# FFT filter and two MLPs on one core: six of sixteen units turned by 64x64 products, filters in places of their own, and the last reload cut in two

## What is computed

```
X = rfft(x, axis=1); y = irfft(X * (filt_r + 1j * filt_i), n=3008, axis=1)
x = y.reshape(6016, 256)
h = x @ w1_in;  x = max(0.01 * h, h) @ w1_out        # 256 -> 2048 -> 256
h = x @ w2_in;  out = max(h, 0)**2 @ w2_out
```

## Time and profile before

| | |
|---|---|
| median of 3 runs | 1065.8 us (1065.09 to 1067.39) |
| the profiled execution | 1064.64 us, of which the span is 1062.5 us |
| PE busy | 1057.0 us, 99% of the span |
| DVE, ACT, POOL busy | 827.9, 563.3, 316.1 us |
| granted TensorE clock | 1.00 of full speed throughout |
| DMA | 61.45 MB, 58 GB/s over the span, 79% of the share from 20 to 90 us |

### The profile page before, as it was taken

One profiled execution on the slowest core, in us unless ns is written; L12 is line 12 of the kernel. 1 busy time (PEld: TensorE's weight loads), 2 busy tenths in 40 slices (PEclk: granted clock), 3 DMA queues, 4 the chain that ended last, 5 costly groups with the idle time before them and its releaser, 6 DMA issues.

```text
span 1062.5 us, 13988 instructions
## 1 busy us (share of the span) xinstructions
PE 1057.0 (99%) x5120; PEld 879.8 (83%) x5120; DVE 827.9 (78%) x1142; ACT 563.3 (53%) x979; POOL 316.1 (30%) x287
## 2 busy tenths in 40 slices
PE   9999999999999999999999999999999999999998
PEld 9558888888888888888999888888888888888998
DVE  2877898887887887787887886887887887786666
ACT  3667564564554654555554554644554554454543
POOL 1995654434343343341321211220220220210000
PEclk9999999999999999999999999999999999999999
DMA  9696000121112112112344000100100100100100
GB/s 316 176 304 231 10 1 17 36 52 46 51 49 49 52 47 51 52 33 55 118 152 147 21 1 1 40 1 1 40 1 1 40 1 1 40 1 1 40 1 35
DMA packets 66724, 61.45 MB, mean 58 GB/s; under 512 B 40688, under 2 KB 53856, under 8 KB 66656
## 3 DMA queue, kind: packets, MB, share of 16 engines
q1 hardware_dynamic: 66160, 60.06, 18.2%
q10 hardware_dynamic: 496, 0.49, 0.1%
HBM read 36.55 MB, written 23.99 MB: 57 GB/s over the span
## 4 chain that ended last, share of the span: by engine, by line
PE 98%; DMA 1%; SPq 0%; DVE 0%; ACT 0%; issue 0%; ACTq 0%
PE PS L1046 16%; PE PS L1047 16%; PE PS L1048 16%; PE PS L1054 14%; PE PS L1055 14%; PE PS L1056 14%; PE PS L935 2%; PE PS L959 2%; PE PS L1002 1%; PE PS L1022 1%; PE PS L979 1%; DMA X<-in_x 0%; DMA zu<-U 0%; DMA V<-zu 0%; SPq L219 0%; PE PS L999 0%
## 5 line engine op out<-in xcount | busy, mean ns | idle before, releaser
L683 ACT ACTIVATE GH<-GF 128x512 fp32r<-128x512 f32 (+1 forms) x384 | 238.7, 622 | 295.3 <-DVE GF L878 154.4
L884 DVE TENSOR_TENSOR GL<-GF,GH 128x512 fp32r<-128x512 f32 (+1 forms) x384 | 273.7, 715 | 110.4 <-ACT GH L683 103.7
L1048 PE MATMUL PS<-GH,WOL 128*128 128x512 f32 (+1 forms) x768 | 295.8, 385 | 0.0
L1047 PE MATMUL PS<-GL,WOH 128*128 128x512 f32 (+1 forms) x768 | 295.8, 385 | 0.0
L1046 PE MATMUL PS<-GH,WOH 128*128 128x512 f32 (+1 forms) x768 | 295.8, 385 | 0.0
L1054 PE MATMUL PS<-XH,WIH 128*128 128x512 f32 (+1 forms) x672 | 259.5, 386 | 0.0
L1056 PE MATMUL PS<-XH,WIL 128*128 128x512 f32 (+1 forms) x672 | 258.8, 385 | 0.0
L876 DVE SCALAR_TENSOR_TENSOR GF<-GF 128x512 f32<-128x512 f32 (+1 forms) x192 | 167.5, 913 | 1.6
L1048 PEld LDWEIGHTS PS<-GH,WOL 128*128 128x128 f32 x768 | 144.2, 188 | 27.0
L1046 PEld LDWEIGHTS PS<-GH,WOH 128*128 128x128 f32 x768 | 144.2, 188 | 26.8
L1047 PEld LDWEIGHTS PS<-GL,WOH 128*128 128x128 f32 x768 | 144.2, 188 | 26.6
(11 more groups left out here) (85 smaller groups left out, 941.9 us busy)
## 6 DMA issues: line engine op xcount, KB each, us to landing
V<-zu SPq DMA_DIRECT2D x12, 512.0 KB, 5.9
zu<-U SPq DMA_DIRECT2D x31, 192.0 KB, 3.7
out_y<-YT SPq DMA_DIRECT2D x5, 1024.0 KB, 4.3
X<-in_x SPq DMA_DIRECT2D x8, 512.0 KB, 8.9
FL<-in_filt SPq DMA_DIRECT2D x16, 224.0 KB, 5.0
wi<-PWH SPq DMA_DIRECT2D x16, 224.0 KB, 2.5
wi<-PWL SPq DMA_DIRECT2D x16, 224.0 KB, 3.1
WIH<-wi SPq DMA_DIRECT2D x8, 448.0 KB, 3.4
```

Of the source, the lines that this page charges most:

```text
L683: nc.scalar.activation(GH[:, g, 0:width(s)], GF[:, g, 0:width(s)], ACT.Copy).then_inc(g_hi[kind], 1)
L884: nc.vector.tensor_tensor(GL[:, g, 0:w], GF[:, g, 0:w], GH[:, g, 0:w].bitcast(f32), ALU.subtract).then_inc(g_lo[kind], 1)
L1047: nc.tensor.matmul(acc, wh, xl, start=False, stop=False)
L1048: return nc.tensor.matmul(acc, wl, xh, start=False, stop=last)
```

## The change

1. **Turn by quarters.** In units 4, 6, 8, 10, 12 and 14 (`by_quarters`), the turn is no longer 8 transposes but 32 ordinary products with the 64x64 identity: for each sequence and frequency, two halves of the feature rows times two halves of the output columns (rows 0 to 47 and 64 to 111 of the result). Bank 0 now takes the first 64 features and bank 1 the last 64, for both sequences, so ACT copies only once all of it is done. In those units the turn stands ahead of `spectrum` in the pass.
2. **Filters.** Each of the 16 filters has a place of its own, ten of them (FLA) in WIH's room behind group 1, six (FLB) where FL was. SP no longer waits for DVE to load them, and loads the weight groups w1i 3 to 6 earlier. In return the rounding of group 2 moves on DVE to behind the last copy of U, and its sums on POOL from units 8 and 11 to behind the units, together with group 3's.
3. **V's second half.** Rows 0 to 95 (units 8 to 13) are loaded by ACT in three DMAs once those units are stored, right behind `x_round0(1)`; rows 96 to 127 (units 14 and 15) by SP in three DMAs once all is stored. The pieces are 4, 8 and 12 of 24 column groups.
4. **PE's order.** `up_1(1)` moves to right behind `up_1(0)`, ahead of sequence 12.

```diff
+V_PIECES = ((0, 4), (4, 12), (12, 24))
+V_BODY = 96
-FSLOTS = 6
+F_EARLY = 10
...
+        def by_quarters(i):
+            return i >= 4 and i % 2 == 0
...
             def load_filter(i):
-                if i >= FSLOTS:
-                    sp.wait_ge(prod, 3 * (i - FSLOTS + 1))
-                elif i == 0:
+                if i == F_EARLY:
                     for half in range(2):
                         sp.wait_ge(n1_ps[half], CH // 2)
...
+            for n in range(3):
+                sp.wait_ge(p_ps, 4 * n + 4)
+                load_filter(6 + n)
+                if n < 2:
+                    load_w1i(3 + n)
             for i in range(UNITS):
-                if i + FSLOTS < UNITS:
-                    load_filter(i + FSLOTS)
                 store_u(i)
-                if i in (1, 2, 4, 6):
-                    load_w1i(WI_EARLY + (1, 2, 4, 6).index(i))
+                if 9 + i < UNITS:
+                    load_filter(9 + i)
+                if i in (1, 2):
+                    load_w1i(4 + i)
...
             for n in range(UNITS - RINGS, UNITS):
                 sp.wait_ge(*stored(n))
-            for g in range(MH // 4):
-                load_v(1, g)
+            for n in range(len(V_PIECES)):
+                load_v_rest(n)
...
-                if i in (8, 11):
-                    wi_sums(2, (8, 11).index(i))
...
+            for k in (2, 3):
+                for part in range(2):
+                    wi_sums(k, part)
             for part in range(3):
-                wi_split(WI_EARLY - 1, part)
-            for k in range(WI_EARLY, WI_SEAM):
+                wi_split(2, part)
+            for k in (4, 5, 6):
                 for part in range(2):
                     wi_sums(k, part)
...
             def turned(i):
+                if by_quarters(i):
+                    act.wait_ge(s2_ps, turned_steps(i + 1))
+                    for h in range(2):
+                        nc.scalar.activation(S2[:, i % 2, :, :, 64 * h:64 * h + 64].rearrange("p b j d -> p (b j) d"),
+                                             PS[0:KR, h, :].rearrange("p (n d) -> p n d", d=64), ACT.Copy).then_inc(s2_sb, 1)
...
             def wi_round(k):
                 act.wait_ge(wi_s, 4 * k + 4)
+                act.wait_ge(wi_hi, k)
...
                 if c == 4:
                     x_round0(1)
+                    for n in range(UNITS - 2 - RINGS, UNITS - 2):
+                        act.wait_ge(z_out[n % RINGS], 32 * (n // RINGS + 1))
+                    for n in range(len(V_PIECES)):
+                        load_v_body(n)
...
-            wi_round(WI_EARLY - 1)
             back(UNITS - 2)
             dve.wait_ge(yf_sb, 2 * UNITS)
             y_copy(1)
             back(UNITS - 1)
+            wi_round(2)
...
+                        for h in range(2):
+                            d = slice(64 * h, 64 * h + 64)
+                            c = 64 * (UJ * b + k)
+                            for part in range(2):
+                                mm = nc.tensor.matmul(PS[IM * part:IM * part + R, h, c:c + 64], TT1[half][d, b, q + part, 0:R],
+                                                      DM[d, 2, d], start=True, stop=True)
...
             for i in range(UNITS):
+                if i + 3 < UNITS and by_quarters(i + 3):
+                    turn(i + 3)
                 if i + 2 < UNITS:
                     spectrum(i + 2)
-                if i + 3 < UNITS:
+                if i + 3 < UNITS and not by_quarters(i + 3):
                     turn(i + 3)
...
             up_1(0)
+            up_1(1)
             for c in range(CH, 19):
```

More of the change, by code:

```diff
@@ L50, in fft_mlp_kernel @@
     BF = [at(f"BF{r}", [KR, 2, B, 2 * 128], f32, (8, 0, 4)[r] * KB) for r in range(RINGS)]
-    FL = at("FL", [KR, FSLOTS, 2, 2 * 128], f32, 12 * KB)
+    FLA = at("FLA", [KR, F_EARLY, 2, 2 * 128], f32, o_wi + 7 * KB)
+    FLB = at("FLB", [KR, UNITS - F_EARLY, 2, 2 * 128], f32, 12 * KB)
+    FL = [FLA[:, i, :, :] if i < F_EARLY else FLB[:, i - F_EARLY, :, :] for i in range(UNITS)]
     U = at("U", [KR, RINGS, UJ, B * 128], f32, 36 * KB)
@@ L104, in fft_mlp_kernel @@
         warm_sb = sem("warm_sb")
-        ft_in = [sem(f"ft_in{g}") for g in range(FSLOTS)]
+        ft_in = [sem(f"ft_in{i}") for i in range(UNITS)]
         tw_in = sem("tw_in")
@@ L117, in fft_mlp_kernel @@
         z_out = [sem(f"z_out{r}") for r in range(RINGS)]
-        v_in = [[sem(f"v_in{h}{g}") for g in range(MH // 4)] for h in range(2)]
+        v_in = [sem(f"v_in{g}") for g in range(MH // 4)]
+        v_body = [sem(f"v_body{n}") for n in range(len(V_PIECES))]
+        v_rest = [sem(f"v_rest{n}") for n in range(len(V_PIECES))]
         y_ps = sem("y_ps")
@@ L209, in drained, with turned_steps @@
             return range(DRAIN[n], DRAIN[n + 1])
+        def by_quarters(i):
+            return i >= 4 and i % 2 == 0
+        def turned_steps(i):
+            return sum(4 if by_quarters(n) else 2 for n in range(i))
         def wo_slot(k):
@@ L249, in stored, with load_v, load_v_rest @@
                 return z_out[i % RINGS], 32 * (i // RINGS + 1)
[L251 to L254, removed]
+            def load_v(g):
+                by_js = zu[0].rearrange("j s m e -> (j s) m e")
+                sp.dma_start(V[0][:, 4 * g:4 * g + 4, :, :].rearrange("p m b d -> p m (b d)"),
+                             by_js[:, 4 * g:4 * g + 4, :]).then_inc(v_in[g], 16)
+            def load_v_rest(n):
+                a, b = V_PIECES[n]
+                by_js = zu[1].rearrange("j s m e -> (j s) m e")
+                sp.dma_start(V[1][V_BODY:, a:b, :, :].rearrange("p m b d -> p m (b d)"), by_js[V_BODY:, a:b, :]).then_inc(v_rest[n], 16)
             for b in range(B):
@@ L263, in _ @@
             load_w1i(1)
-            for i in range(FSLOTS):
+            for i in range(6):
                 load_filter(i)
@@ L543, in turned @@
             def turned(i):
-                for b in range(B):
-                    act.wait_ge(s2_ps, 2 * i + b + 1)
-                    nc.scalar.activation(S2[:, i % 2, b, :, :].rearrange("p j d -> p (j d)"), PS[0:KR, b, :], ACT.Copy).then_inc(s2_sb, 1)
+                if by_quarters(i):
[3 more added lines that the diff above has]
+                                             PS[0:KR, h, :].rearrange("p (n d) -> p n d", d=64), ACT.Copy).then_inc(s2_sb, 1)
+                else:
+                    for b in range(B):
+                        act.wait_ge(s2_ps, turned_steps(i) + b + 1)
+                        nc.scalar.activation(S2[:, i % 2, b, :, :].rearrange("p j d -> p (j d)"), PS[0:KR, b, :], ACT.Copy).then_inc(s2_sb, 1)
             def back(i):
@@ L1007, in sequence @@
                 half, g, b = c // CH, c % CH // 2, c % 2
-                pe.wait_ge(v_in[half][g], 16)
+                if half == 0:
+                    pe.wait_ge(v_in[g], 16)
+                else:
+                    piece = [a <= 4 * g < b for a, b in V_PIECES].index(True)
+                    pe.wait_ge(v_body[piece], 16)
+                    pe.wait_ge(v_rest[piece], 16)
                 if c == 0:
@@ L1159, in _ @@
             for s in range(1, SLOTS):
-                up_1(s)
-                if s == 1:
+                if s > 1:
+                    up_1(s)
+                else:
                     sequence(22)
```

31 lines of the change are left out of this document (21 added, 10 removed).

## The result

| | before | after |
|---|---|---|
| median | 1065.44 us (1064.16 to 1067.39, 6 runs) | 1072.84 us (1070.2 to 1075.65, 6 runs) |
| ratio, 95% interval | | 1.0067 [1.0054, 1.008] |
| profiled execution | 1064.64 us, span 1062.5 | 1073.25 us, span 1071.1 |

The forecast was 1065.4 us, no change, with a range to 1067.3. The time lies 5.5 us outside it.

A forecast was written before the change was run, and what follows sets the result against it. PE bounds the kernel, busy 1057.0 of 1062.5 us. Terms -1.7 + 0.4 + 0.4 + 1.0 - 0.7 + 0.2 = -0.4 us take 1064.64 to 1064.2; the median, 1.2 above, gives 1065.4, range 1063.4 to 1067.3.

The forecast's parts named there:

- V's second half: Behind the units: smaller last loads may start sequence 12 up to 1.7 us sooner; nothing lasting, bounds 0 and 0.5 us won.
- The rival on V: From about 80 us, ACT's body of V holds up the stores: up to +0.2 us, 1066.0, or 1067.3; chance 0.15.
- a fall of the clock: Sign of error, whole run: the forecast is wrong if the clock, 1.00 before throughout, falls.
- The quarter turn: In the units: 0.90 us against 1.18 for eight transposes, saving 0.28 us each, 1.7 us for six.
- Weights can't be changed that fast: Slower rival, in the units: a quarter turn takes 1.76 us, +3.5 us in all, 1069.8 us; chance 0.07.
- PE's waits for POOL: In the units: 0.4 us for the latency of DVE and POOL and 0.4 us for POOL's remainders.
- What the units won: By the last inverse: PE ahead by 1.7 us of turns less 0.8 of waits, 0.9 us.
- the move of the sums: Group 2's sums leave units 8 and 11, where they were hidden; claimed to win nothing there.
- The late copies: Behind the units: group 2's sums delay ACT's copies and `x_split0(2)`, so `up_2(0)` waits; +1.0 us.
- ACT's rounding of group 6: Behind the units: begins 1.95 us later for group 2's sums, less 0.9, at about 87.6 us.
- `up_1(1)`: Ahead of sequence 12: fills 0.7 of PE's 1.2 us wait for V, so -0.7 us.
- `group_d(0)`: At about 102 us: PE waits for DVE's later sum, 0.2 us more.

The follow-up runs named there:

- split_rows: The kernel before, with each of the six loads of V's second half cut into rows 0 to 95 and 96 to 127, all on SP: 1067.71 us.
- v_whole: The changed kernel, with V's second half loaded as before, six loads of 128 rows on SP once every unit is stored: 1065.29 us, ratio 0.9993.
- one_queue: The changed kernel, but SP issues V's body of 96 rows too, ahead of the waits for the last stores: 1073.99 us, ratio 1.0078.
- body_one_piece: The changed kernel, but ACT loads only the body's first piece, SP the rest of that piece and five whole groups: 1065.15 us, ratio 0.9998.
- quarters_only: The kernel before with the quarter turns alone; filters, V and PE's order as before: 1064.91 us, ratio 0.9995.
- quarters_early_up: The kernel before with the quarter turns and `up_1(1)` early; filters, sums and V as before: 1064.16 us, ratio 0.9995.
- best_of_all: The kernel before with quarter turns, `up_1(1)` early, and V's second half's first 512 KB cut into rows 0 to 95 (ACT) and 96 to 127 (SP): 1064.54 us.
- long_rows: The kernel before, with V's second half in three loads of 128 rows, of 4, 8 and 12 groups, all on SP: 1066.02 us, ratio 1.0005.
- first_group_last: The kernel before, with the group of V's second half that sequence 12 needs first loaded last: 1074.35 us, ratio 1.0084.

## Why the prediction was wrong

**The step that failed is "V's second half".** I booked it at 0, with bounds of 0 and 0.5 us won, reasoning that its last loads carry 128, 256 and 384 KB rather than six times 512. Three things are wrong in it.

- *What stands ahead.* The rest's first 128 KB came behind the body, 2.25 MB for all column groups, most of which sequence 12 doesn't need. The kernel before had one idle stretch to put a body in: 82 to 84 us at 26 GB/s. Two microseconds at 390 GB/s hold 0.8 MB. That row I had not read; the one I used, 80 to 81 us at 323 GB/s, said that there is no room before. The rival on V had the place right and the size wrong: it let the body delay the stores (they were on time, 4.6 us, landing at 83.7), where it was the body that delayed the rest.
- *The rate.* I took the full rate for loads of 96 and 32 rows. They run at 188 to 270 GB/s. In a good order this costs 2.3 us (split_rows), in the change's order more: by 84 us some 0.6 MB of the body is in (packet records), and 1.9 MB are left to the end of the rest's first piece. At 390 GB/s these take 4.9 us, at the 230 seen here 8.3. By this estimate the rate makes 3.4 us of the wait, and at the full rate sequence 12 would still have started near 88.9 us, 2.1 later than before. It is rough: at 230 GB/s it ends at 92.3 us, and 93.51 was measured. The body ahead of the rest at the full rate was not run in just this form.
- *The clock.* Behind its 6.7 us without work PE was granted 0.50 until about 98 us. I had named a fall of the clock as a sign of error, but priced it in no rival. It is 2.5 of the 8.6 us between the two profiled executions.

**What held.** The quarter turn: 0.90 us forecast, 0.90 and 0.91 measured; with the inverses behind it at 0.92 a pair of units takes 5.56 us (5.52 forecast, 5.80 before). "Weights can't be changed that fast" fell, and with it the 25 ns from start to start that the prediction cites from the Trainium skill (TensorE: Matmul & The Clock Gate, "Wait — 56ns, not 53.3ns?"): 64 records in 0.90 us are 14 ns for each. PE's waits for POOL came to 1.0 us, where 0.8 was booked. What the units won in all is less clear. The four profiles with the change's units (after, v_whole, one_queue, body_one_piece) need 52.59, 52.80, 52.09 and 51.56 us, mean 52.26; of nine with the old units five take 52.66 or 52.67, the longest 54.06, mean 53.03. By the means that is 0.8 us against the 0.9 forecast, against the five it is 0.4, and the spread from one execution to the next is larger than either. With the sums of group 2 left in the units (quarters_only, quarters_early_up, best_of_all) the mean is 52.8, from 51.95 to 53.24. That may mean that the move of the sums, which I had said wins nothing, carries the gain; these profiles don't show it. The late copies: forecast to hold `up_2(0)` at about 93.1, measured 93.79 with DVE's wait of 0.8 once V was out of the way; in the change itself V's lateness hid them, and the copy of sequence 12 waited 4.9 us for PE:

```profile
89.72 0.95 ACT L594 ACTIVATE WIH<-WIF 128x896 fp32r<-128x896 f32 x1 [0.94 <-POOL WIF L385]
95.59 0.60 ACT L589 ACTIVATE YT<-PS 128x512 f32<-128x512 f32 x1 [4.92 <-PE PS L1079]
```

ACT's rounding of group 6 was due at 87.6 and came at 89.7, 3.1 us later than before: 1.9 by group 2's sums, 0.55 since POOL ended its last unit that much later, and the rest mostly by POOL itself, whose remainders of group 2 took longer than the 2.37 us of before:

```profile
80.72 3.27 POOL L391 TENSOR_TENSOR WIL<-WIF,WIH 128x384 fp32r<-128x384 f32 x3
```

So the term of 1.0 us for the late copies was too small as well: in body_one_piece `up_2(0)` came 0.75 us later than before although the last inverse came 0.69 sooner, 1.4 in all. `up_1(1)` was forecast at -0.7, with 0.2 given back at `group_d(0)`; -0.6 and 0.3 were measured. Without the step on V, the forecast (1065.4) is what v_whole measured (1065.29). That it fits so closely is in part luck: the units won somewhat less and the copies cost 0.4 more than booked, PE still waited 1.65 us for V in v_whole, and the forecast started from a median of 1065.8 where the kernel before had 1065.39 beside v_whole.

## What to carry to other kernels

Cut a transfer by what its first reader needs, not by what is ready: a piece sent early helps only if it fits into idle time of the queues, and that time has a row of its own to be read. In these runs a load's rate depended on which rows of the tile it covers; cut along the free dimension, or across row 64, before cutting the rows. Where a forecast contains a wait of PE of several microseconds, price the slower clock behind it too.

## What was not expected of the hardware

- Over two microseconds, loads of rows 0 to 63 ran at 207 to 234 GB/s, of rows 0 to 95 at 256 to 272, of rows 96 to 127 at 212, of all 128 at 360 to 430 (86 to 92 us of before, long_rows and first_group_last); 96 and 32 rows in turn gave 233 to 246. Over single microseconds rows 32 to 95 ran at 303 to 393 in loads of 512 KB, and at 197 to 311 in loads of 256 KB, with gaps.
- Loads that another engine issued later on its own queue moved nothing for 5 us while earlier ones of ACT's queue were left.
- The 32 products of a quarter turn, 64 records, fill 0.90 us: 14 ns per record, each with its own load of weights.
